# One masked sum over experts, an eleventh weight segment, and a one-hot product with swapped sides in an attention and double mixture kernel

## The reference, cut to what matters

```python
x = chunked attention of q, k, v and 8 memory slots        # (3072, 512)
# first mixture: 8 experts with 4 slots each
logits = x @ phi                                            # (3072, 32)
slot_input = softmax over tokens(logits).T @ x              # (32, 512)
for e in range(8):
    slot_out[e] = np.maximum(slot_input[e] @ w1m[e], 0) @ w2m[e]    # w1m[e] 512x1024, w2m[e] 1024x512
x = softmax over slots(logits) @ slot_out                   # = combine @ slot_out
# second mixture: each token goes to one expert
e_idx = argmax(x @ w_gate, axis=1)
out[mask] = gate * eom * (np.maximum(x[mask] @ w1[e], 0) @ w2[e])
```

## Time and profile before

| | |
|---|---|
| median of three runs | 552.07 us (548.39 to 554.98) |
| the profiled execution's own time | 552.02 us |
| its span | 550.3 us |
| mean granted TensorE clock | 0.934 of full |
| PE busy | 481.5 us, 88% of the span |
| DVE, ACT, POOL busy | 213.0, 201.1, 135.6 us |
| moved by the transfers | 97.89 MB |
| attention until the last partial sum | about 0 to 182.3 us |
| slot stage until the last weights of it | to 239.8 us |
| routing and first gathers | to 288.2 us |
| tiles | to 541 us |

### The profile page before, as it was taken

How to read it: one execution, slowest core, us unless ns; L and a number is a source line. 1 busy time by engine, 2 the same in 40 slices (tenths; PEclk the granted TensorE clock), 3 DMA queues, 4 the chain that set the end, 5 groups by cost and what they waited for, 6 DMA issues and landing times.

```text
span 550.3 us, 11392 instructions
## 1 busy us (share of the span) xinstructions
PE 481.5 (88%) x3728; PEld 282.7 (51%) x3729; DVE 213.0 (39%) x974; ACT 201.1 (37%) x769; POOL 135.6 (25%) x128
## 2 busy tenths in 40 slices
PE   3789989988988797687839999999999999999993
PEld 3677767777766232344824444444444444444441
DVE  3677778777875420017522121221222122212210
ACT  1799898899896111110000111111111111111110
POOL 2244334333433010000521121212221222122210
PEclk9799999999999598975658999999999999999998
DMA  9989999999993999999993817851110111010000
GB/s 152 186 174 256 190 248 268 194 253 270 198 239 137 335 324 324 339 366 369 381 401 125 320 26 247 272 190 41 41 39 21 41 41 39 22 41 3 2 0 0
DMA packets 122416, 97.89 MB, mean 178 GB/s; under 512 B 95680, under 2 KB 96176, under 8 KB 122384
## 3 DMA queue, kind: packets, MB, share of 16 engines
q1 hardware_dynamic: 115600, 77.70, 52.3%
q10 hardware_dynamic: 3168, 12.58, 6.5%
q0 software_dynamic: 3616, 7.20, 3.9%
HBM read 90.78 MB, written 8.52 MB: 180 GB/s over the span
## 4 chain that ended last, share of the span: by engine, by line
PE 72%; DMA 13%; DVE 8%; issue 3%; ACT 1%; POOL 1%; SPq 0%; ACTq 0%; POOLq 0%; DVEq 0%
PE bank L765 40%; DMA arena<-in_moe_w_dram 11%; PE bank L520 7%; PE bank L589 5%; PE bank L749 4%; DVE arena L837 3%; PE bank L535 3%; PE bank L731 2%; PE bank L565 2%; PE bank L545 2%; PE bank L718 2%; PE bank L599 1%; PE bank L548 1%; PE bank L559 1%; DMA arena<-rows_scratch,tok_sorted 1%
## 5 line engine op out<-in xcount | busy, mean ns | idle before, releaser
L765 PE MATMUL bank<-arena 128*128 x496 | 226.4, 604 | 0.0
L765 PEld LDWEIGHTS bank<-arena 128*128 128x128 f32 x496 | 90.4, 192 | 103.9 <-issue 100.4
L455 POOL TENSOR_TENSOR arena<-arena,row_inv 96x1024 f32<-96x1024 f32 x32 | 60.6, 1893 | 108.0 <-DVE row_inv L830 108.0
L488 POOL DMA_INDIRECT out_dram<-arena,tok_sorted x31 | 31.4, 1013 | 195.1 <-ACT arena L1147 195.1
L1016 DVE TENSOR_SCALAR arena<-bank 128x256 f32<-128x256 f32 x124 | 44.0, 418 | 63.9 <-PE bank L749 63.9
L1147 ACT ACTIVATE arena<-bank,gate_sorted 128x512 f32<-128x512 f32 x31 | 21.3, 687 | 103.6 <-PE bank L765 103.6
L837 DVE CUSTOM_DVE_ANT_0 arena<-bank,masks 96x128 f32<-96x128 f32 x256 | 55.1, 277 | 3.3 <-PE bank L520 3.3
L1140 ACT COPY arena<-bank 128x128 f32<-128x128 f32 x31 | 8.2, 266 | 118.7 <-PE bank L740 118.7
L1049 ACT ACTIVATE arena<-arena,neg_max 96x128 f32<-96x128 f32 x128 | 49.9, 398 | 2.3 <-issue 1.5
L1058 ACT ACTIVATE arena<-arena,neg_max 96x128 f32<-96x128 f32 x128 | 49.8, 394 | 0.0
L520 PE MATMUL bank<-shared 64*96 64x128 f32 x512 | 37.6, 287 | 11.6 <-issue 6.1
(11 more groups left out here) (161 smaller groups left out, 525.8 us busy)
## 6 DMA issues: line engine op xcount, KB each, us to landing
arena<-in_moe_w_dram SPq DMA_DIRECT2D x26, 2048.0 KB, 10.8
arena<-in_moe_w_dram ACTq DMA_DIRECT2D x6, 2048.0 KB, 10.5
arena<-in_k_dram SPq DMA_DIRECT2D x32, 240.0 KB
arena<-in_v_dram SPq DMA_DIRECT2D x32, 240.0 KB
arena<-in_q_dram SPq DMA_DIRECT2D x32, 192.0 KB
arena<-in_mem_k_dram SPq DMA_DIRECT2D x32, 16.0 KB
arena<-in_mem_v_dram SPq DMA_DIRECT2D x32, 16.0 KB
arena<-rows_scratch,tok_sorted POOLq DMA_INDIRECT x31, 3.5
```

Of the source, the lines that this page charges most:

```text
L455: g.tensor_tensor(probs[:, t % 4], probs[:, t % 4], row_inv[:, t % 2, :].unsqueeze(2).to_broadcast([TQ, H, NK]), ALU.mult).then_inc(p_norm ...
L488: pool.indirect_dma_start(out=out, out_offset=bass.IndirectOffsetOnAxis(ap=tok_sorted[:, j:j + 1].bitcast(U32), axis=0), in_=o_sb[:, j % 2 ...
L765: ins = mm(bank[4 + par][:, :], h_t[:, par, f * 128:(f + 1) * 128], w2_all[:, bass.ds(e * SEG + f * DM, DM)], start=(f == 0), stop=(f == K ...
```

## The change

It has these parts.

- The arena gets an eleventh segment; seven w1m matrices are early ones (PRE = 7). The seventh is issued by ACT in the first drain step of attention. `k_t`, `q_t`, `x_t` and the routing's tables move to other places in memory.
- The order of the transfers becomes all w1m, then all w2m, then w1[0] to w1[4], w2[0], w1[5] to w1[7], w2[1] to w2[7].
- DVE multiplies each relu by a column of zeros and ones (`own_slots`), so that only the rows of a slot's own expert stay. All eight `down` then sum in one bank; one ACT copy and one product with `fold` of 32 columns take the place of eight copies and eight `pick`.
- The one-hot product takes `spots` (now 64 wide) as stationary and `hot_tok` (128 wide) as moving operand, even tiles into the upper, odd ones into the lower 64 rows of bank 2. A DVE copy and a further product with `fold2` add the halves and turn the result over. DVE, not POOL, multiplies by the token number; POOL multiplies by the gate in two pieces.
- `hidden(3)` and `hidden(4)` move from the first two tiles to behind the one-hot product; the copies of g move from DVE to ACT.

```diff
-    RING = 10
+    RING = 11
-    PRE = 6
+    PRE = 7
-    EARLY_G = 2
+    EARLY_G = 4
+    BEFORE_HOT = 3
+    SPAN = 32
...
+    units = [("up", e) for e in range(E)] + [("down", e) for e in range(E)]
...
+    units += [("hidden", e) for e in range(EARLY_G + 1)] + [("w2", 0)]
+    units += [("hidden", e) for e in range(EARLY_G + 1, E)] + [("w2", e) for e in range(1, E)]
...
                 elif i == PRE + 1:
+                    sp.wait_ge(p_turned, NT)
+                elif i == PRE + 2:
                     sp.wait_ge(weighted, NT)
-                    sp.wait_ge(logit_made, QUADS)
-                    sp.wait_ge(x_turned, NT)
-                elif i == PRE + 2:
-                    sp.wait_ge(p_turned, NT)
...
             for j in range(LAG + TPB * (B - 1), NT + LAG):
                 step(None, j)
+                e = EARLY * (B - 1) + j - LAG - TPB * (B - 1)
+                if e < PRE:
+                    dst, src = matrix(("up", e))[::-1]
+                    act.dma_start(dst, src).then_inc(early_in, 16)
...
-                        ins = mm(bank[6 + e % 2][32 * m:32 * m + NS, :], hid_t[:, e // 2 % 2, at:at + NS],
-                                 w[:, 4 * half + m, :], start=(half == 0), stop=(half == 1))
+                        ins = mm(bank[6][32 * m:32 * m + NS, :], hid_t[:, e // 2 % 2, at:at + NS],
+                                 w[:, 4 * half + m, :], start=(e == 0 and half == 0), stop=(e == E - 1 and half == 1))
...
-                vec.tensor_scalar(hid_rows[:, pr % 2, :], bank[3 + pr % 2][:, :], 0.0, None, ALU.max).then_inc(relu_made, 1)
-            dve.wait_ge(folded, E)
+                vec.tensor_scalar(hid_rows[pr % 2], bank[3 + pr % 2][:, :], 0.0, own_slots[:, pr:pr + 1],
+                                  ALU.max, ALU.mult).then_inc(relu_made, 1)
+            dve.wait_ge(folded, 1)
...
+                    lo = 2 * SPAN * (n % 2)
+                    ins = mm(bank[2][lo:lo + 2 * SPAN, 0:TR], spots[:, n].rearrange("p a j -> p (a j)"),
+                             hot_tok[:, i % 2, t, :], start=(n < 2), stop=(n >= NT - 2))
                 ins.then_inc(hot_used, 1)
+
+            pe.wait_ge(fold2_made, 1)
+            pe.wait_ge(hot_summed, 1)
+            mm(bank[1][:, 0:2 * SPAN], hot_sum, fold2, start=True, stop=True).then_inc(sorted_made, 1)
+            for e in range(BEFORE_HOT, EARLY_G + 1):
+                hidden(e)
...
+            link(vec.tensor_tensor(spots[:, :, 1, :], r_one[:, 6, :].unsqueeze(2).to_broadcast([TQ, NT, SPAN]),
+                                   tile_no[:].unsqueeze(1).to_broadcast([TQ, NT, SPAN]), ALU.is_equal))
+            vec.tensor_tensor(spots[:, :, 0, :], spots[:, :, 1, :],
+                              token_no[:].unsqueeze(2).to_broadcast([TQ, NT, SPAN]), ALU.mult).then_inc(spot_found, 1)
...
+            for e in range(EARLY_G + 1):
+                g_copy(e)
             act.wait_ge(tiles_known, 1)
             pick(0)
             pick(1)
```

More of the change, by code:

```diff
@@ L189, in build @@
         small = tail[:, 2 * F + 2 * DM:]
+        hot_tok = tail[0:TQ, 0:2 * HOT * TR].rearrange("p (r t c) -> p r t c", r=2, t=HOT)
+        routing = tail[0:TQ, 2 * F:2 * F + 2 * DM]
+        r_a = routing[:, 0:NT * E].rearrange("p (t e) -> p t e", t=NT)
+        r_b = routing[:, NT * E:2 * NT * E].rearrange("p (t e) -> p t e", t=NT)
+        r_tiles = routing[:, NT * E:NT * E + E * (N // TR)].rearrange("p (e k) -> p e k", e=E)
+        r_hot = routing[:, 2 * NT * E:3 * NT * E].rearrange("p (e t) -> p e t", e=E)
+        r_rank = routing[:, 3 * NT * E:4 * NT * E].rearrange("p (e t) -> p e t", e=E)
+        r_le = small[0:1, 0:NR * E].rearrange("p (j e) -> p j e", j=NR)
         g_sel = small[:, 0:2 * GF].rearrange("p (r c) -> p r c", r=2)
@@ L465, in _ @@
             pool.dma_start(c_dram[N:N + 1], blank[:]).then_inc(c_out, 16)
+            pool.wait_ge(x_turned, NT)
+            g.memset(fold2, 0.0).then_inc(fold2_part, 1)
+            for r in range(2):
+                pool.wait_ge(fold2_part, r + 1)
+                ins = g.affine_select(out=fold2, in_=fold2, compare_op=ALU.not_equal, fill=1.0, base=-2 * SPAN * r,
+                                      pattern=[[-1, 2 * SPAN]], channel_multiplier=1)
+                ins.then_inc(fold2_part, 1)
+            pool.wait_ge(fold2_part, 3)
+            pool.sem_inc(fold2_made, 1)
             pool.wait_ge(spot_found, 1)
             pool.wait_ge(gate_ready, 1)
-            for i in range(NT // HOT):
-                at = slice(i * HOT, (i + 1) * HOT)
-                g.tensor_tensor(spots[:, at, 1, :], spots[:, at, 0, :],
-                                r_one[:, 1, at].unsqueeze(2).to_broadcast([TQ, HOT, NR]), ALU.mult).then_inc(gate_spread, 1)
-                pool.wait_ge(gate_spread, i + 1)
-                g.tensor_tensor(spots[:, at, 0, :], spots[:, at, 0, :],
-                                token_no[:, at].unsqueeze(2).to_broadcast([TQ, HOT, NR]), ALU.mult).then_inc(spots_made, 1)
+            for i in range(2):
+                at = slice(i * NT // 2, (i + 1) * NT // 2)
+                g.tensor_tensor(spots[:, at, 1, :], spots[:, at, 1, :],
+                                r_one[:, 1, at].unsqueeze(2).to_broadcast([TQ, NT // 2, SPAN]), ALU.mult).then_inc(gate_spread, 1)
             def gather(j):
@@ L720, in hidden @@
                 ins.then_inc(g_made, 1)
-            for e in range(EARLY_G + 1):
+            for e in range(BEFORE_HOT):
                 hidden(e)
@@ L805, in _ @@
             dve.wait_ge(consts_made, CONSTS)
+            for half in range(2):
+                link(vec.tensor_reduce(own_slots[64 * half:64 * half + 64, :],
+                                       fold[64 * half:64 * half + 64, :].rearrange("p (r a b) -> p r a b", a=2, b=SPE)[:, :, half, :],
+                                       AX.X, ALU.add))
             vec.memset(slot_acc, 0.0).then_inc(parts_added, 1)
@@ L1120, in _ @@
                 sc.copy(hid_t[:, pr % 2, :], bank[5][:, :]).then_inc(hid_copied, 1)
[L1121 to L1125 removed]
+            act.wait_ge(down_made, E)
+            sc.copy(out_parts[:, 0, :], bank[6][:, :]).then_inc(down_copied, 1)
             act.wait_ge(ct8_turned, 1)
@@ L1129, in _ @@
             act.wait_ge(gate_shifted, 1)
[L1130 removed]
+            sc.activation(r_a, r_a, ACT.Exp).then_inc(gate_exped, 1)
             act.wait_ge(gate_shifted, 2)
```

189 lines of the change are left out of this document (87 added, 102 removed).

## The result

The changed kernel takes **535.48 us** (median of four runs, 533.35 to 540.63) where the kernel before took 551.62; the ratio is 0.974, 95% interval 0.9694 to 0.9786. The forecast was 538, with a range of 531 to 546. The profiled execution took 533.35 with a span of 531.6, so it is 2 us quicker than its median; the profiled execution of before, 552.02, stood at its median. Of the 18.7 us between the two spans some are therefore the executions' own. Three traces of the changed kernel and two of the one before, all further down, tell which. Medians leave out executions in the chip's slower state, one of 540.39 us and one of 555.12.

A forecast was written before the change was run, and what follows sets the result against it. Tiles bound by PE, slot stage by its weights, the stretch between by latency; −6.4 + 1.1 − 3.9 − 1.2 − 3.7 = −14.1 against 552.02 gave 538 us, range 531 to 546.

The forecast's parts named there:

- part 2: Slot stage's weights: earlier first w2m, one matrix fewer, 2 us dry spell; last weights land at 233.4, −6.4 us.
- part 1: Attention's drain: ACT issues one more matrix on the path, +0.4 us.
- part 3: From last weights to gate logits: pick removed, copy added, fold and `down` perhaps at low clock; +1.1, from −0.2 to +3.7.
- part 4: Routing up to the one-hot product: gate ready 0.5 later, POOL's first piece 3.0 beside DVE; product starts +0.5 us.
- part 5: One-hot product with sides swapped takes 7.0 us, −5.5; copy and summing product add +0.9; together −4.6.
- Rival (c): One-hot product: no overlap between column halves, 5.5 us given back; kernel at 543 us, chance 0.05.
- part 6: Start of the tiles: gather path (280.1) and PE with ACT (280.2) tie; −3.9 us for parts 4 to 6.
- part 7: Clock at the tiles' start: two dense `hidden` closer by may raise it for L765's first half tile; −1.2, 0 to −3.6.
- part 8: Tiles: two `hidden` of 1.86 us each leave, −3.7 us; the g copies on ACT cost nothing.
- (a): Low clock at slot stage's end, one-hot product and `hidden`, dry spell costing double: 546 us, chance 0.13.
- (b): No dry spell in the transfer queue and a high clock: 530 us, chance 0.10.
- (d): Slower: first tile waits for w2[1] if its expert is 1; 548 to 561 us, 554, chance 0.03.

The follow-up runs named there:

- all eight traces: Three traces of the changed kernel and five of variants changing something behind its slot stage, that stage untouched: 47.8 us on average for the stage.

## Why the prediction was right, and where it was not

**The weights (part 2)** were the largest term and the one mis-sized: −6.4 forecast, −11.8 between the two profiles, −9.6 by the means, −8.1 with all eight traces. The wait for the first `up`, five matrices behind it instead of six, and the early issue all came as said. Two things were off. The base trace's pace, 6.03 us a w2m, is at the slow end of what these kernels show; the second trace of the kernel before has 5.4, the changed one (228.03 − 205.66) / 4 = 5.6. And the 2 us of restart were not paid in full. The first `up` released its issue at 193.53 (before 194.76); it began 0.4 us earlier (187.90, 188.34), and the granted clock from 192 to 196 us was 1.00, where it had been 0.77. The third w2m was then still arriving (the next issue, released by its landing, is at 195.91), and the share of 0.71 in those 4 us makes about 1.2 us of pause. The bound of −8.9 stood for no dry spell at all. What the sum did not say is that the two parts are worth much less one by one.

**The drain (part 1).** PE's rows of the drain stand 0.35 us later from the first ACT issue on (the product that began at 174.99 before began at 175.34), where 0.4 was said. It is lost in attention's end, which varies by 4.6.

**From the weights to the gate logits (part 3):** +1.1 forecast, +1.2 by the means. `down(6)` took 3.57 and `down(7)` 1.92 in the first trace, 3.64 for `down(7)` in the second: the clock at that point is a matter of the execution, as the range from −0.2 to +3.7 allowed.

**To the one-hot product (part 4):** +0.5 forecast, −0.4 measured, in every trace. The gate was ready 0.55 later, as said (POOL began 11.78 us behind the gate logits, before 11.23). But PE could start 2.2 us after POOL's first piece began, not 3.0. The step that failed is the reading of the earlier trace rows, a slowdown in proportion to the elements. The instructions one by one, each in its own view:

```profile
249.79 1.22 DVE L1014 TENSOR_TENSOR arena<-r_one,lane_no 96x1024 f32<-96x1024 f32 x1
249.87 2.05 POOL L490 TENSOR_TENSOR token_side<-token_side,r_one 96x512 f32<-96x512 f32 x1 [52.01 <-DVE r_one L1005]
250.94 2.06 DVE L1014 TENSOR_TENSOR arena<-r_one,lane_no 96x1024 f32<-96x1024 f32 x1
251.89 2.02 POOL L490 TENSOR_TENSOR token_side<-token_side,r_one 96x512 f32<-96x512 f32 x1
```

The ends are 251.01, 251.92, 253.00 and 253.91, 0.9 to 1.1 us apart, DVE and POOL in turn: each row's length holds the other engine's turn. The earlier trace rows has the same: POOL's 96x248 piece of 1.44 us ended 0.47 behind the end of DVE's first L984 (261.81), so it was 0.97 of waiting and 0.47 of work. Read so, a wait of 1.1 us and twice the 0.47 would have given 2.0 us for the first piece. This agrees with the exclusive lock of the Trainium skill (SBUF — State Buffer, "SBUF: two separate sides"), which one engine holds for the whole of an instruction while the other is blocked. The prediction had weighed it as a wait for both of DVE's pieces, and the rows show a wait for one. What it took for evidence against the lock, that POOL's pieces begin in the middle of DVE's stretch, tells only when a row begins, not when it works.

**The one-hot product (part 5):** −4.6 with its summing product forecast, −3.8 by the means (−3.0 to −5.2). L589 was the right row to go by, 0.055 against the 0.065 measured at the high clock. The rule of the Trainium skill (TensorE: Matmul & The Clock Gate, "Part 3"), that weight loads overlap running matmuls only across row groups, does not predict this by itself: both products use the same 96 rows, and alternating halves of the columns took the pass from 0.115 to 0.065. The same section also has a row for matmuls packed side by side in the columns ("3× col (M=32, N=512)", 2.38×), and that is the kind of case that came; the prediction left it out. Rival (c) is ruled out by the 0.065. The copy and the summing product cost 1.2, not 0.9.

**The start of the tiles (parts 6 and 7).** The tie was there, and ACT decided it: +0.8 on the way from gather to product, where parts 4 to 6 left +0.2 for it (the whole of them came to −3.4, against −3.9). In the first trace PE idled 1.73 us for `ct_copy` before that product. The prediction had named a new wait for ACT at this place as a sign of being wrong: in two traces of three it came, at the price of about 1 us, and the third has 6.7 us as before the change. In two of three traces ACT waited 2.6 and 4.0 us before its last g copy for something that the trace calls unknown. The clock's −1.2 did not come: the first half tile took 5.26, 5.14 and 6.3 us, before 6.00 and 4.70. PE was still idle for 2.25 us until the gathered rows were spread (2.07 and 4.36 in the other traces), and the granted clock was 0.53 from 270.1 to 274.0. This was the step that was wrong in kind, of small size.

**The tiles (part 8):** −3.7 forecast, −3.5 measured.

**The rivals.** (a) and (b) were the ends of the range; what came is weights near those of (b) (−8.9, against −8.1 to −9.6), without the clock's gain at the start of the tiles. (d) could not happen to the first tile at all: `steps128` begins with −1, so that each expert has at least one tile, and tile 0 is always expert 0's. That could have been read in the kernel.

By the means of three traces the errors are −3.2 (weights), +0.1 (part 3), −0.9 (part 4), +0.8 (part 5), +0.6 (part 6), +1.0 (part 7) and +0.2 (part 8), −1.4 in sum. That 535.48 came so near to 538 is in part luck: too small a gain in the weights was offset by a clock gain that did not come and by the tiles' start, and the weights' own error lies within what that stage varies by.

## What to carry to other kernels

Find the wait in a queue of transfers that depends on computation, and count the bytes before and behind it. Parts that each keep such a queue ahead of the wait need not be additive: undone alone they cost at most 2.7 us of the stage here, together about 10, some 4 of which may be the pace of that execution. Take the pace of transfers from several executions before pricing a term by it; here it went from 5.4 to 6.2 us for the same 2 MiB. For a small fp32 product like this one, make the narrow operand stationary and alternate between column halves. Where two engines' rows stretch each other, look at the single instructions and their ends before taking a ratio.

## What the runs showed of the hardware that was not expected

Two 2 MiB transfers in flight ran at 5.4 us each in one execution and at 5.1 and 7.5 in turn in another, same program, same matrices.

Alternating column halves sped up an fp32 pass of 64 stationary and 128 moving columns from 0.115 to 0.065 us at the high clock, on the same rows; at the low clock it took 0.115 alternating.

DVE's 96x1024 and POOL's 96x512 products, running beside each other, ended in turn, 0.9 to 1.1 us apart. None waited for two instructions of the other engine.

ACT stood still for 2.6 to 4.0 us before a copy whose operand had been complete for 1.8 to 3.3 us, in five of the eleven traces with `hidden(4)` ahead of the tiles. Its cause stays open; no run here was made to find it.
